# A chunked recurrence with two expert layers on one Trainium2 core: the triangular inverse in two interleaved streams, its solve on four 32x32 tiles, and later loads of the first layer's weights

## The chip, the cores and the metric

One core of a Trainium2 chip runs the whole program. The metric is the device time of one execution in microseconds. The kernel before takes 1128.68 us (median of 3 runs, 1117.59 to 1130.25).

## The reference, cut to what matters

```python
for t in range(S):                                   # S = 768 steps, 4 batches x 8 heads, D = 40
    y[:, :, t] = np.einsum('bhd,bhde->bhe', rt, state)
    Sa = np.einsum('bhde,bhe->bhd', state, at)
    state = state * wt[:, :, None, :] - np.einsum('bhd,bhe->bhde', Sa, bt)
    state = state + np.einsum('bhd,bhe->bhde', vt, kt)
x = y as 3072 tokens x 320
x = leaky(x @ w_in) @ w_out                          # 320 -> 2048 -> 320
out = (sigmoid(x @ w_gate) * (x @ w_val)) @ w_out2   # 320 -> 1536 -> 320
```

All of it is float32. The steps of one head depend on each other, the heads don't.

## The kernel before, in words

**The recurrence.** The 768 steps are cut into chunks of L = 64. A unit is 2 chunks (c = 0, 1) of 16 heads; there are NU = 12 units, and 24 pairs n = 2u + c. Eight heads lie beside each other in the free dimension (q = 0 to 7) and two more on the two halves of the partitions (i = 0, 1). Inside a chunk the sequential part is a unit lower triangular system. Its 64x64 matrix is split at C = 32 into two diagonal 32x32 blocks and one 32x32 cross block. All 64 diagonal blocks of a unit are inverted at once on VectorE: they are written to DRAM (`store_p`), come back with one block to each partition in `p_unit` (`load_p_top`, `load_p_low`: rows 0 to 15 and 16 to 31; two half inverses of each block lie on 128 partitions), and `inverse_columns` builds the inverse in `t_unit` column by column. A column is one multiply (L1255, into `prod`) and one add (L1259), over t//2 + 1 rows by 31 - t elements; each waits for the one before by a semaphore. The inverse goes back over DRAM (`store_t`, `load_t`) into `t_sb`.

**A pair n on TensorE** (PE), with the engine that empties each result: `pe_rhs_begin/end` (right side; ScalarE, `act_rhs`), `pe_first` (L698, upper half of the solve: `t_sb` times `rhs_sb`, 16 matmuls of 32x32 by 40; ScalarE, `act_first`), `pe_cross` (L708, the upper half's part in the lower half; ScalarE, `act_cross`), `pe_a_ka` (L630, L636: the matrices of unit g + 2 and g + 1; `act_a`, which also copies the cross block into `p_cross`, and `dve_ka`), `pe_ut_u` (L744, L747), `pe_st` (L761, the new state; VectorE, `dve_st`), `pe_vrur`, `pe_y_begin_sn`, `pe_y_end`. `pe_first` and `pe_cross` use the tile positions of the upper half of each i only. `FILL` lists matmuls with no use (L897) that stand behind some of these steps in the first units; 56 of them stand ahead of the first `pe_first`.

**Order.** Nothing is scheduled by a planner: each engine runs a hand-written loop over windows g = -2, -1, 0, ... and steps s = 0 to 7; unit g is in its main part in window g. From g = 2, s = 2 on, step number m = 8g + s - 18 of the first expert layer stands in each s: `up_products(m)` (L811), `act_g`, `dve_g_low` (L1306) and `down_products(m - 1)` (L826 to L831). There are 96 such steps, and then 72 steps of the second layer (L861, L879 to L881), which have TensorE alone from about 650 us on. In each window VectorE works at 31 columns: of unit g + 1 columns 7 to 12 at s = 0, 13 to 19 at s = 3, 20 to 26 at s = 4, 27 to 30 at s = 5, and of unit g + 2 columns 0 to 6 at s = 7.

**Weights of layer 1** come in 8 pieces of 0.6 to 0.8 MB into four staging buffers: GpSimd issues them (`load_piece`), ScalarE rounds them (`split_hi`), VectorE computes what is left over (`split_lo`, L1332 to L1339). Pieces 0 to 3 are issued at the end of window -1. GpSimd's queue also holds the products of a, b, k with the decays (`pool_a`, `pool_b`, `pool_k`) and the fetches of the next a, b, k. SyncE's queue holds nearly all other transfers, in the order of `sync_program`.

## Time and profile before

| | |
|---|---|
| runs, us | 1117.59, 1128.68, 1130.25 |
| profiled execution, us | 1121.75 (span of the profile 1120.0) |
| busy share | TensorE 94%, weight loads 80%, VectorE 55%, ScalarE 35%, GpSimd 13% |
| mean granted clock of TensorE | 0.98 of full speed |
| chain that ended last | TensorE 83%, VectorE 7%, issue 4%, the rest 6% |

The span is the stretch from the first to the last instruction, and the profiled execution took 1.75 us more than it. A matmul that overlaps with its neighbours has a long record, so TensorE's busy share doesn't say how much it achieved; the starts of its instructions do. "Idle before" names what ended an engine's wait.

### The profile page before, as it was taken

The numbers are of one execution on the slowest core, as the hardware profiler recorded it, in microseconds if no ns is written. First come the engines' busy times: TensorE is split into PE (matmuls) and PEld (weight loads), VectorE is DVE, ScalarE is ACT, GpSimd is POOL, SyncE is SP. The second block draws the span as 40 slices with busy tenths as digits, with TensorE's granted clock in tenths as the row PEclk, the third lists the DMA queues.
The fourth block names the chain that finished last, engine by engine and source line by source line (L and its number), as shares of the span: only waits on it lengthen the run. The fifth ranks groups of instructions, "written<-read, shape, count | busy, mean of one in ns | idle before, by whom it ended". The sixth has DMA issues, their size and how long they took to land.

```text
span 1120.0 us, 36607 instructions
## 1 busy us (share of the span) xinstructions
PE 1053.4 (94%) x16106; PEld 897.1 (80%) x16106; DVE 612.3 (55%) x1330; ACT 397.6 (35%) x782; POOL 145.1 (13%) x179
## 2 busy tenths in 40 slices
PE   3887779999999999999999999999999999999998
PEld 2776668788787877787878788888888888888887
DVE  7788977768687777677664234343232232323222
ACT  2142334345344443433443345542222222222222
POOL 6313130312213130303000000000000000000000
PEclk9988979999999999999999999999999999999999
DMA  5936364343426342533433034230202002020000
GB/s 176 256 93 153 87 123 94 88 111 107 116 47 142 88 110 61 132 81 93 96 84 76 9 106 135 77 90 1 61 1 62 1 1 62 1 61 1 24 1 23
DMA packets 133857, 87.63 MB, mean 78 GB/s; under 512 B 98274, under 2 KB 113634, under 8 KB 133700
## 3 DMA queue, kind: packets, MB, share of 16 engines
q1 hardware_dynamic: 126740, 62.85, 23.1%
q0 software_dynamic: 6960, 22.45, 6.8%
q8 instruction: 127, 2.08, 0.8%
q14 instruction: 30, 0.25, 0.1%
HBM read 66.39 MB, written 18.87 MB: 76 GB/s over the span
## 4 chain that ended last, share of the span: by engine, by line
PE 83%; DVE 7%; issue 4%; ACT 2%; POOL 2%; DMA 1%; SPq 0%; ACTq 0%; DVEq 0%; POOLq 0%
PE bank L811 15%; PE bank L861 12%; PE pair L861 12%; PE bank L881 4%; PE bank L879 4%; PE bank L880 4%; PE bank L826 4%; PE bank L827 3%; PE bank L828 3%; DVE prod L1255 2%; DVE t_unit L1259 2%; PE bank L786 2%; PE bank L630 2%; PE bank L897 2%; PE bank L830 2%
## 5 line engine op out<-in xcount | busy, mean ns | idle before, releaser
L1306 DVE TENSOR_TENSOR g_lo<-g_full,g_hi 128x512 fp32r<-128x512 f32 x168 | 125.2, 745 | 208.9 <-ACT g_hi L1066 208.8
L1066 ACT CAST g_hi<-g_full 128x512 fp32r<-128x512 f32 x168 | 104.4, 621 | 135.0 <-DVE g_full L1359 132.0
L811 PE MATMUL bank<-x_hi,w_up 128*128 128x512 f32 x480 | 135.8, 413 | 0.4 <-issue 0.2
L1059 ACT ACTIVATE g_full<-bank 128x512 f32<-128x512 f32 x96 | 57.5, 599 | 197.2 <-PE bank L811 185.9
L1255 DVE TENSOR_TENSOR prod<-t_unit,p_unit 128x126 f32<-128x126 f32 (+22 forms) x372 | 99.5, 267 | 19.8 <-DMA p_unit<-p_dram 6.5
L1259 DVE TENSOR_TENSOR t_unit<-t_unit,prod 128x126 f32<-128x126 f32 (+22 forms) x372 | 102.2, 275 | 12.8
L811 PEld LDWEIGHTS bank<-x_hi,w_up 128*128 128x128 f32 x480 | 86.0, 190 | 19.7 <-issue 0.9
L1359 DVE TENSOR_TENSOR g_full<-pair,h_sb 128x512 f32<-128x512 f32 x36 | 24.9, 691 | 113.1 <-PE pair L861 112.4
L811 PE MATMUL bank<-x_lo,w_up 128*128 128x512 f32 x288 | 82.0, 393 | 0.0
L826 PE MATMUL bank<-g_hi,w_dn 128*128 128x512 f32 x192 | 77.2, 402 | 2.9 <-DVE g_lo L1306 2.9
L1359 DVE TENSOR_TENSOR g_full<-bank,h_sb 128x512 f32<-128x512 f32 x36 | 24.9, 691 | 94.3 <-PE bank L861 86.3
L827 PE MATMUL bank<-g_hi,w_dn 128*128 128x512 f32 x192 | 75.1, 391 | 0.0
L828 PE MATMUL bank<-g_lo,w_dn 128*128 128x512 f32 x192 | 74.9, 390 | 0.0
L811 PEld LDWEIGHTS bank<-x_lo,w_up 128*128 128x128 f32 x288 | 54.7, 190 | 12.3
L861 PE MATMUL bank<-x_hi,up 128*128 128x512 f32 x240 | 62.8, 391 | 0.0
L861 PE MATMUL pair<-x_hi,up 128*128 128x512 f32 x240 | 62.8, 391 | 0.0
L630 PE MATMUL bank<-a_sb,b_sb 40*64 40x64 f32 x768 | 34.2, 252 | 28.2 <-POOL a_sb L301 24.9
L881 PE MATMUL bank<-dn,g_lo 128*128 128x320 f32 x192 | 59.3, 309 | 0.0
L880 PE MATMUL bank<-dn,g_hi 128*128 128x320 f32 x192 | 59.3, 309 | 0.0
L879 PE MATMUL bank<-dn,g_hi 128*128 128x320 f32 x192 | 59.1, 308 | 0.0
L630 PEld LDWEIGHTS bank<-a_sb,b_sb 40*64 40x64 f32 x768 | 30.7, 163 | 30.6 <-issue 26.1
L861 PEld LDWEIGHTS bank<-x_hi,up 128*128 128x128 f32 x240 | 44.1, 188 | 7.9
(149 smaller groups left out, 2410.7 us busy)
## 6 DMA issues: line engine op xcount, KB each, us to landing
p_unit<-p_dram SPq DMA_DIRECT2D x48, 128.0 KB, 2.9
stage<-in_w_out POOLq DMA_DIRECT2D x7, 640.0 KB, 5.0
v_tok<-in_vT SPq DMA_DIRECT2D x12, 320.0 KB, 3.2
v_nu<-in_vN SPq DMA_DIRECT2D x24, 160.0 KB, 5.6
x<-y_sb SPq DMA_DIRECT2D x48, 80.0 KB
k_sb<-in_kF POOLq DMA_DIRECT2D x22, 160.0 KB, 3.4
v_sb<-in_vF SPq DMA_DIRECT2D x22, 160.0 KB
r_sb<-in_rF SPq DMA_DIRECT2D x22, 160.0 KB
```

What stands on the lines that cost most here:

```text
L811: last = nc.tensor.matmul(up_bank(m)[:], lhs, rhs, start=(e == 0), stop=(e == len(products) - 1))
L826: nc.tensor.matmul(bank[1 + kk][:], w_high, hi, start=(f == 0), stop=False)
L827: nc.tensor.matmul(bank[1 + kk][:], w_low, hi, start=False, stop=False)
L828: nc.tensor.matmul(bank[1 + kk][:], w_high, lo, start=False, stop=(f == NF1 - 1))
L861: last = nc.tensor.matmul(o[:], lhs, rhs, start=(x == 0), stop=(x == len(products) - 1))
L879: nc.tensor.matmul(o, g_hi[:, par, tok], wt[:, 0, f % GT], start=(f == 0), stop=False)
L880: nc.tensor.matmul(o, g_hi[:, par, tok], wt[:, 1, f % GT], start=False, stop=False)
L881: last = nc.tensor.matmul(o, g_lo[:, par, tok], wt[:, 0, f % GT], start=False, stop=(f == NF2 - 1))
L1066: nc.scalar.copy(g_hi[:, m % 2], g_full[:]).then_inc(g_hi_ready, 1)
L1255: nc.vector.tensor_tensor(terms, t_unit[:, 0:m, t:t + 1].to_broadcast([P, m, rest]), p_unit[:, t, t + 1:C].unsqueeze(1).to_broadcast([P, m ...
L1259: nc.vector.tensor_tensor(t_unit[:, 0:m, t + 1:C], t_unit[:, 0:m, t + 1:C], terms, ALU.add).then_inc(column_ready, 1)
L1306: nc.vector.tensor_tensor(g_lo[:, m % 2], g_full[:], g_hi[:, m % 2].bitcast(F32), ALU.subtract).then_inc(g_lo_ready, 1)
```

## The change

It has seven parts.

- `inverse_columns` handles a column as two streams, the even and the odd rows of `t_unit`, each with its own semaphores: multiply even, multiply odd, add even, add odd. `columns_done` waits for both.
- From g = 2 on the columns of unit g + 1 lie otherwise: 7 to 10 at s = 0, 11 to 13 at s = 2, 14 to 19 at s = 3; the rest as before.
- `pe_first` writes heads q < 4 to the upper and q >= 4 to the lower quarter of each half, and `pe_cross` reads them there. The order of q is 0, 4, 1, 5, ..., so four 32x32 tile positions come in turn. `act_a` copies `p_cross` in four pieces in place of two.
- Pieces 0 to 3 of the weights are issued in window 0, behind `pool_a` of unit 2 and a wait for `t_loaded` of unit 0.
- `split_hi` of pieces 0 to 3 lies one step later in window 0 (s = 1 to 4), `split_lo` too (s = 3 to 6).
- SyncE issues `load_p_top(1)` ahead of `store_t(0)`.
- ScalarE runs `act_first` ahead of `act_x` in even windows.

```diff
@@ pool
+                if g == 0:
+                    pool.wait_ge(t_loaded, 64)
+                    for i in range(4):
+                        load_piece(pool, i)
                 if g == 1:
                     load_piece(pool, 6)
...
-                if g == -1:
-                    pool.wait_ge(p_low_loaded, 32)
-                    for i in range(4):
-                        load_piece(pool, i)
@@ SyncE
+            load_p_top(sp, 1)
             store_t(sp, 0)
-            load_p_top(sp, 1)
@@ TensorE, pe_first and pe_cross
-            for q in range(TQ):
+            for q in (x for low in range(HQ) for x in (low, low + HQ)):
                 for i in range(2):
-                    last = nc.tensor.matmul(o[upper(i), q * D:(q + 1) * D], t_sb[upper(i), c, q, 0:C],
+                    last = nc.tensor.matmul(o[first_rows(i, q), q * D:(q + 1) * D], t_sb[upper(i), c, q, 0:C],
                                             rhs_sb[upper(i), q], start=True, stop=True)
...
-                    last = nc.tensor.matmul(rhs_place(q)[lower(i)], p_cross[upper(i), u % 2, c, q],
-                                            u_first[upper(i), q], start=False, stop=True, skip_group_check=True)
+                    last = nc.tensor.matmul(rhs_place(q)[lower(i)], p_cross[first_rows(i, q), u % 2, c, q],
+                                            u_first[first_rows(i, q), q], start=False, stop=True,
+                                            skip_group_check=True)
@@ ScalarE
+                    if s == 1 and now:
+                        act_first(act, n)
                     if s == (0 if g == NU else 1) and g % 2 == 0 and 2 <= g // 2 <= NJ:
                         act_x(act, g // 2 - 1)
...
-                    if g == 0 and s < 4:
-                        split_hi(act, s)
+                    if g == 0 and 1 <= s <= 4:
+                        split_hi(act, s - 1)
@@ VectorE, inverse_columns
+                for e in range(min(m, 2)):
+                    rows = (m + 1 - e) // 2
+                    terms = prod[:, 80 * e:80 * e + rows * rest].rearrange("p (r t) -> p r t", t=rest)
+                    streams.append((e, rows, terms))
+                for e, rows, terms in streams:
+                    wait(dve, column_ready[e], done[e])
+                    nc.vector.tensor_tensor(terms, t_unit[:, e:m:2, t:t + 1].to_broadcast([P, rows, rest]),
+                                            p_unit[:, t, t + 1:C].unsqueeze(1).to_broadcast([P, rows, rest]), ALU.mult
+                                            ).then_inc(column_multiplied[e], 1)
+                for e, rows, terms in streams:
+                    dve.wait_ge(column_multiplied[e], done[e] + 1)
+                    nc.vector.tensor_tensor(t_unit[:, e:m:2, t + 1:C], t_unit[:, e:m:2, t + 1:C], terms, ALU.add
+                                            ).then_inc(column_ready[e], 1)
@@ VectorE, vector_program
-                        inverse_columns(dve, g + 1, 7, 13)
+                        inverse_columns(dve, g + 1, 7, 11 if g >= 2 else 13)
+                    elif s == 2 and soon and g >= 2:
+                        inverse_columns(dve, g + 1, 11, 14)
                     elif s == 3 and soon:
-                        inverse_columns(dve, g + 1, 13, 20)
+                        inverse_columns(dve, g + 1, 14 if g >= 2 else 13, 20)
...
-                    if g == 0 and 2 <= s <= 5:
-                        split_lo(dve, s - 2)
+                    if g == 0 and 3 <= s <= 6:
+                        split_lo(dve, s - 3)
```

The order on VectorE in a window from g = 2 on, from the decay of step 1 to the first columns of step 3 (`u_first` and `st_sb` are the state's update, `x_f` the two results of `pe_vrur`; a row ends with partitions x elements). Before:

```order
L1240 SCALAR_TENSOR_TENSOR inv<-w_raw,restart 128x520
L1306 TENSOR_TENSOR g_lo<-g_full,g_hi 128x512
L1275 TENSOR_TENSOR u_first<-pair,st_sb 128x320
L1278 TENSOR_TENSOR st_sb<-u_first,decay 128x320
L1288 TENSOR_TENSOR x_f<-bank,mask 128x512 x2
L1255 TENSOR_TENSOR prod<-t_unit,p_unit 128x126
L1259 TENSOR_TENSOR t_unit<-t_unit,prod 128x7x18
L1255 TENSOR_TENSOR prod<-t_unit,p_unit 128x136
L1259 TENSOR_TENSOR t_unit<-t_unit,prod 128x8x17
```

And now:

```order
L1257 SCALAR_TENSOR_TENSOR inv<-w_raw,restart 128x520
L1278 TENSOR_TENSOR prod<-t_unit,p_unit 128x60 x2
L1283 TENSOR_TENSOR t_unit<-t_unit,prod 128x3x20 x2
L1278 TENSOR_TENSOR prod<-t_unit,p_unit 128x76
L1278 TENSOR_TENSOR prod<-t_unit,p_unit 128x57
L1283 TENSOR_TENSOR t_unit<-t_unit,prod 128x4x19
L1283 TENSOR_TENSOR t_unit<-t_unit,prod 128x3x19
L1278 TENSOR_TENSOR prod<-t_unit,p_unit 128x72
L1278 TENSOR_TENSOR prod<-t_unit,p_unit 128x54
L1283 TENSOR_TENSOR t_unit<-t_unit,prod 128x4x18
L1283 TENSOR_TENSOR t_unit<-t_unit,prod 128x3x18
L1330 TENSOR_TENSOR g_lo<-g_full,g_hi 128x512
```

Columns 11 to 13 (elements 20, 19 and 18 long) have moved ahead of `g_lo`, and each column has four rows where it had two.

GpSimd's queue from the last products of window -1 on. Before:

```order
L301 TENSOR_TENSOR a_sb<-a_sb,decay 128x512
L329 DMA stage<-in_w_in 128x1536
L331 DMA stage<-in_w_out 128x1280
L329 DMA stage<-in_w_in 128x1536 x2
L438 DMA k_sb<-in_kF 40x1024 x2
L429 DMA b_sb<-in_bF 40x1024 x2
L321 TENSOR_TENSOR k_sb<-k_sb,inv 128x512
L311 TENSOR_TENSOR b_sb<-b_sb,inv 128x512
L301 TENSOR_TENSOR a_sb<-a_sb,decay 128x512
L420 DMA a_sb<-in_aF 40x512 x2
```

And now:

```order
L307 TENSOR_TENSOR a_sb<-a_sb,decay 128x512
L444 DMA k_sb<-in_kF 40x1024 x2
L435 DMA b_sb<-in_bF 40x1024 x2
L327 TENSOR_TENSOR k_sb<-k_sb,inv 128x512
L317 TENSOR_TENSOR b_sb<-b_sb,inv 128x512
L307 TENSOR_TENSOR a_sb<-a_sb,decay 128x512
L335 DMA stage<-in_w_in 128x1536
L337 DMA stage<-in_w_out 128x1280
L335 DMA stage<-in_w_in 128x1536 x2
L426 DMA a_sb<-in_aF 40x512 x2
```

The four weight loads have moved behind the fetches of k and b and three products, and the fetch of a now stands behind them.

ScalarE in an even window from g = 4 on, step 1. Before:

```order
L1066 CAST g_hi<-g_full 128x512
L1076 CAST x_hi<-x_f 128x512 x3
L1023 COPY u_first<-bank 128x320
L1030 COPY rhs_sb<-pair 128x160 x2
L981 ACTIVATE p_sb<-bank 128x512
L983 ACTIVATE p_cross<-bank 32x256 x2
```

And now:

```order
L1082 CAST g_hi<-g_full 128x512
L1039 COPY u_first<-bank 128x320
L1092 CAST x_hi<-x_f 128x512 x3
L1046 COPY rhs_sb<-pair 128x160 x2
L994 ACTIVATE p_sb<-bank 128x512
L997 ACTIVATE p_cross<-bank 32x128 x4
```

The copy that `pe_cross` waits for has moved ahead of three casts, and `p_cross` is written in four copies of half the size.

## Rows read from the trace of the kernel before

**Rows 1.** Four stretches: us, busy time of each engine, PEclk, DMA share, GB/s

```profile
25.00:55.00 30.00, 25.27 (x404) 24.29 (x404) 21.35 (x78) 6.15 (x14) 10.17 (x14) 1.00 0.92 256
55.00:65.00 10.00, 9.78 (x207) 9.08 (x208) 7.18 (x21) 3.53 (x10) 0.00 (x0) 0.52 0.08 23
...
100.00:150.00 50.00, 37.25 (x1131) 33.16 (x1130) 43.93 (x105) 16.47 (x35) 14.14 (x18) 0.84 0.61 133
...
200.00:300.00 100.00, 97.72 (x2260) 80.24 (x2254) 75.39 (x184) 43.86 (x95) 20.47 (x26) 1.00 0.43 103
```

**Rows 2.** The chain that ended last, near the first solve: start us, us, what

```profile
37.19 14.90 PE bank L897 x112
52.09 3.13 issue
55.22 1.15 PE bank L698 x32
```

**Rows 3.** SyncE's issues, 29 to 52 us: start us, us, line, transfer

```profile
28.97 15.33 SPq L477 DMA_DIRECT2D p_dram<-p_sb  x8
44.34 3.07 SPq L504 DMA_DIRECT2D t_dram<-t_unit  x2
...
49.97 2.17 SPq L515 DMA_DIRECT2D t_sb<-t_dram  x4
```

**Rows 4.** Transfers issued from 25 to 60 us: size, us from issue to landing

```profile
stage<-in_w_in POOLq DMA_DIRECT2D x3, 768.0 KB, 13.6
...
t_dram<-t_unit SPq DMA_DIRECT2D x2, 128.0 KB, 4.8
t_sb<-t_dram SPq DMA_DIRECT2D x4, 64.0 KB, 3.5
```

**Rows 5.** VectorE, two dependent instructions of the inverse of unit 0

```profile
36.10 0.29 DVE L1255 TENSOR_TENSOR prod<-t_unit,p_unit 128x126 f32<-128x126 f32 x1
36.43 0.29 DVE L1259 TENSOR_TENSOR t_unit<-t_unit,prod 128x126 f32<-128x126 f32 x1
```

**Rows 6.** VectorE, neighbours of which neither waits for the other

```profile
68.15 1.27 DVE L1288 TENSOR_TENSOR x_f<-bank,mask 128x512 f32<-128x512 f32 x2
...
75.94 1.39 DVE L1299 TENSOR_TENSOR y_sb<-bank,decay 64x512 f32<-64x512 f32 x2
...
77.70 1.22 DVE L1339 TENSOR_TENSOR w_dn<-stage,w_dn 128x1024 fp32r<-128x1024 f32 x1
78.84 0.28 DVE L1255 TENSOR_TENSOR prod<-t_unit,p_unit 128x121 f32<-128x121 f32 x1
```

**Rows 7.** VectorE, the state updates of pairs 0, 1, 2 and 3

```profile
66.37 0.49 DVE L1275 TENSOR_TENSOR u_first<-pair,st_sb 128x320 f32<-128x320 f32 x1 [0.97 <-PE pair L761]
...
87.13 0.49 DVE L1275 TENSOR_TENSOR u_first<-pair,st_sb 128x320 f32<-128x320 f32 x1
...
112.84 0.49 DVE L1275 TENSOR_TENSOR u_first<-pair,st_sb 128x320 f32<-128x320 f32 x1 [2.02 <-PE pair L761]
...
131.36 0.49 DVE L1275 TENSOR_TENSOR u_first<-pair,st_sb 128x320 f32<-128x320 f32 x1
```

**Rows 8.** TensorE in windows 6 and 7: start us, us, line, matmul, idle before

```profile
353.88 0.76 PE L698 MATMUL bank<-rhs_sb,t_sb 32*32 32x40 f32 x32
354.57 0.50 PE L826 MATMUL bank<-g_hi,w_dn 128*128 128x512 f32 x1
...
359.17 0.42 PE L630 MATMUL bank<-a_sb,b_sb 40*64 40x64 f32 x3 [0.86 <-POOL a_sb L301]
...
411.09 0.27 PE L630 MATMUL bank<-a_sb,b_sb 40*64 40x64 f32 x2
...
412.07 0.23 PE L744 MATMUL pair<-t_sb,rhs_sb 64*40 64x64 f32 x2
```

**Rows 9.** Waits over the whole span: us in total, times, longest

```profile
PE pair L708 <- ACT u_first L1023: 3.1, 4, 1.1
...
PE bank L826 <- DVE g_lo L1306: 2.9, 3, 1.0
```

More of the change, by code:

```diff
@@ L105, in rwkv_mlp_kernel @@
         t_unit = sb(ctx, "t_unit", [P, C // 2, C])
-        prod = sb(ctx, "prod", [P, 136])
+        prod = sb(ctx, "prod", [P, 152])
         def vrur(i):
@@ L160, in rwkv_mlp_kernel @@
         diagonal_set = sem("diagonal_set")
-        column_multiplied = sem("column_multiplied")
-        column_ready = sem("column_ready")
+        column_multiplied = [sem(f"column_multiplied{i}") for i in range(2)]
+        column_ready = [sem(f"column_ready{i}") for i in range(2)]
         t_stored = sem("t_stored")
@@ L202, in lower, with first_rows @@
             return slice(L * i + C, L * i + 2 * C)
+        HQ = TQ // 2
+        def first_rows(i, q):
+            return upper(i) if q < HQ else lower(i)
         def wait(engine, signal, value):
@@ L488, in load_p_top @@
                 if u > 0:
-                    sp.wait_ge(column_ready, (C - 1) * (u - 1) + C // 2)
+                    columns_done(sp, u - 1, C // 2)
                 load_p_rows(sp, slice(0, C // 2), p_top_loaded)
@@ L493, in load_p_low, with columns_done @@
             if unit_in(u):
-                wait(sp, column_ready, (C - 1) * u)
+                if u > 0:
+                    columns_done(sp, u - 1, C - 1)
                 load_p_rows(sp, slice(C // 2, C), p_low_loaded)
+        def columns_done(engine, u, t):
+            wait(engine, column_ready[0], (C - 1) * u + t)
+            wait(engine, column_ready[1], (C - 3) * u + t - 2)
         def store_t(sp, u):
             if unit_in(u):
-                sp.wait_ge(column_ready, (C - 1) * (u + 1))
+                columns_done(sp, u, C - 1)
                 wait(sp, t_loaded, 64 * u)
@@ L705, in pe_cross @@
             emptied(pe, "first", n)
-            for q in range(TQ):
+            for q in (x for low in range(HQ) for x in (low, low + HQ)):
                 for i in range(2):
-                    last = nc.tensor.matmul(rhs_place(q)[lower(i)], p_cross[upper(i), u % 2, c, q],
-                                            u_first[upper(i), q], start=False, stop=True, skip_group_check=True)
+                    last = nc.tensor.matmul(rhs_place(q)[lower(i)], p_cross[first_rows(i, q), u % 2, c, q],
+                                            u_first[first_rows(i, q), q], start=False, stop=True,
+                                            skip_group_check=True)
             last.then_inc(cross_multiplied, 1)
@@ L982, in act_a @@
             for i in range(2):
-                last = nc.scalar.mul(p_cross[upper(i), u % 2, c], src[upper(i), :, C:L], -1.0)
+                for q in (0, HQ):
+                    last = nc.scalar.mul(p_cross[first_rows(i, q), u % 2, c, q:q + HQ],
+                                         src[upper(i), q:q + HQ, C:L], -1.0)
             last.then_inc(bank_emptied[bank_of("a", n)], 1)
@@ L992, in act_t_unit @@
             wait(act, t_stored, 32 * u)
-            wait(act, column_ready, (C - 1) * u)
+            if u > 0:
+                columns_done(act, u - 1, C - 1)
             nc.scalar.copy(t_unit[:].rearrange("p r t -> p (r t)"), restart[:, 1:2].to_broadcast([P, C // 2 * C])
@@ L1139, in scalar_program @@
                         act_g(act, m)
+                    now, soon, later = unit_in(g), unit_in(g + 1), unit_in(g + 2)
+                    if s == 1 and now:
+                        act_first(act, n)
                     if s == (0 if g == NU else 1) and g % 2 == 0 and 2 <= g // 2 <= NJ:
                         act_x(act, g // 2 - 1)
-                    now, soon, later = unit_in(g), unit_in(g + 1), unit_in(g + 2)
                     if s == 0 and now:
@@ L1146, in scalar_program @@
                         if now:
-                            act_first(act, n)
                             act_cross(act, n)
@@ L1252, in inverse_columns @@
                 m, rest = t // 2 + 1, C - 1 - t
-                terms = prod[:, 0:m * rest].rearrange("p (r t) -> p r t", t=rest)
-                wait(dve, column_ready, (C - 1) * u + t)
-                nc.vector.tensor_tensor(terms, t_unit[:, 0:m, t:t + 1].to_broadcast([P, m, rest]),
-                                        p_unit[:, t, t + 1:C].unsqueeze(1).to_broadcast([P, m, rest]), ALU.mult
-                                        ).then_inc(column_multiplied, 1)
-                dve.wait_ge(column_multiplied, (C - 1) * u + t + 1)
-                nc.vector.tensor_tensor(t_unit[:, 0:m, t + 1:C], t_unit[:, 0:m, t + 1:C], terms, ALU.add
-                                        ).then_inc(column_ready, 1)
+                done = ((C - 1) * u + t, (C - 3) * u + t - 2)
+                streams = []
+                for e in range(min(m, 2)):
[11 more added lines that the diff above has]
+                                            ).then_inc(column_ready[e], 1)
         def dve_ka(dve, n):
```

## The prediction, as it was put on record before the changed kernel ran

> **What bounds the kernel now.** I read the windows first: between 200 and 300 us TensorE has matmuls running for 97.72 of 100 us [rows 1]. From the first expert layer on, only less TensorE time or fewer of its waits can help. The prologue ahead of it is another matter, so I read the chain there. In it TensorE runs 56 useless matmuls from 37.19 to 52.09, waits 3.13 us, and starts the first solve at 55.22 [rows 2]. What it waits for is the inverse of unit 0. SyncE's issues show how it comes: it is stored from 44.34 and loaded from 49.97, and one batch of eight small stores ahead of it took 15.33 us to issue [rows 3]. The transfers of that stretch tell why: the DMA engines are 92% busy at 256 GB/s [rows 1] while the weight pieces take 13.6 us to land, a store of the inverse 4.8 and its load 3.5 [rows 4]. Right behind the wait the granted clock falls to 0.52 [rows 1], that is from 2.4 GHz to the lower level of 1.2. After that the prologue is paced by VectorE: the state updates of pairs 0 and 1 start 20.8 us apart, those of pairs 2 and 3 18.5 us, and those of pairs 1 and 3 wait for nothing but VectorE's own queue [rows 7].
>
> **Two streams in a column.** Two dependent instructions of 126 elements start 0.33 us apart with 0.29 of work [rows 5]. 1024 elements take 1.22 [rows 6], so an element costs (1.22 - 0.29) / 898 = 1.04 ns, an instruction 0.16 on top, and a dependent successor starts 0.20 plus the elements later. A successor that waits for nothing starts earlier: 1.14 after the 1024 elements (0.08 above their 1.06), and two of 512 take 1.27 together, so the second starts 0.58 after the first (0.05 above 0.53) [rows 6]. A column of 126 costs 2 x 0.33 = 0.66 now. As four instructions of 63 it costs the larger of 4 x (0.066 + 0.08) = 0.58 (the engine) and 2 x (0.066 + 0.20) = 0.53 (the dependence). Short columns gain less; I take 0.075 on each of 29 columns, 2.2 us a unit. Best case, with 0.05 for a start, the dependence rules: 3.5 us gained. Worst case, each instruction pays 0.16 + 0.03 as two neighbours on different halves do (1.39 for two of 64x512, no overlap [rows 6]): 1.02 for that column and about 0.32 lost on each, +9.2 us a unit. I take the middle one since L1255 behind L1339 is the very instruction, with its semaphore already counted up.
>
> The Trainium skill has rules for both sides (VectorE: DVE Perf Modes). Its section "The DRAIN you can't avoid" says that the next operation starts only when the pipe has emptied, and advises few operations, which speaks against this change; the section "Two Vector instructions with no wait between them" says that only neighbours whose operands start in other groups of 32 partitions are held. The rows bear out the second: the overlap is in rows 6, and the pair without one is the pair on two halves. By the first rule the sum would be the slow rival below.
>
> **The start, unit 0.** The store of its inverse is issued at 44.34 [rows 3]; with 2.2 less, 42. Without weights in flight I take 4 us for the store and 4.5 for four issues and the load (landings of 4.8 and 3.5 were under load [rows 4]): 50.5. The useless matmuls last until 52.09, so they cover it by 1.6 us and no more than 3.1 can be had: **-3.1** (bounds 0 and -3.1). The clock: from 55.22 to the state update at 66.37 [rows 2, 7] pass 11.15 us, with solve, filler, `pe_a_ka` and `pe_ut_u` at 1.2 GHz (a solve lasts 1.15 [rows 2], at full clock 0.76 [rows 8]). I assume that without the idle 3.13 us the clock stays up. TensorE's 10 us then become 6, but behind `pe_a_ka` VectorE still has `ka_sb` and a decay (512 elements and two scans of 520 with small steps between, some 3.5 us by my estimate), so 7.5 remain: **-3.7** (bounds 0 and -4.5).
>
> The weights now go out at about 50.5. Landing in 13.6 at worst [rows 4] they are there by 65; rounding them starts behind `pe_ut_u` of pair 0, at about 59, with piece 0, which was issued first. Behind them in GpSimd's queue stand the fetch of a for pair 5 and its product, needed by `pe_a_ka` some 8.5 us after the first state update, near 68: covered by 2 to 3 us. If it is not, that is 2 to 4 us (in the second rival).
>
> **VectorE's stretches.** Between pairs 0 and 1 stand 18 columns (-1.3) and three splits; the third (1024 and 512 elements, so 1.2 + 0.7 us) moves behind the update. That is **-3.1** of 20.8. The row of pair 1 shows no wait for TensorE [rows 7], so it is not next at once; how far ahead it is the row can't tell, which is the near end of the bounds. Between pairs 2 and 3 only the columns are shorter: **-1.3** (bounds for both together: -3.0 and -6.5; with held streams +8). Moving the last split costs nothing: the update of pair 2 comes 25.7 us after that of pair 1 [rows 7], set by the transfers of b and v.
>
> **Steady part, windows 2 to 11.** The solve: 16 matmuls (32 records) take from 353.88 to 354.57, 0.69 us, 0.13 of it to drain: 18 ns a record with two tile positions in use. `pe_a_ka` has four in use: 64 records in 412.07 - 411.09 = 0.98 us, 15 ns each [rows 8]. At 15 a solve takes 0.58, saving 0.11. If tile time alone counted, it would be 18 x 2 / 4 = 9 ns, 0.41 us, saving 0.28. Nearest is `pe_a_ka`; 40 products (`pe_first` and `pe_cross` of 20 pairs) x 0.11 = **-4.4** (bounds 0 and -11). The first four pairs lie in the prologue and count as nothing. The two more copies of `p_cross` cost ScalarE about 0.3 us a pair beside `up_products`: nothing.
>
> Here the skill has an objection (TensorEngine Tiling (Array Packing), "Gotcha 1: PSUM Pressure"): tiles in different rows can't write one PSUM bank at once. `pe_first` writes one bank from both halves of the rows. But so does `pe_a_ka`, at 15 ns [rows 8]; by the rule `pe_first` would save nothing and the sum would be 2.2 higher.
>
> ScalarE's order: `pe_cross` waited for `u_first` 4 times, 3.1 us in all [rows 9], behind three casts of `act_x`. The copy is now first, and the casts lie beside `down_products`. In window 6 `pe_a_ka` waits for GpSimd right after (0.86 [rows 8]), and that wait grows by what is gained: **-2.2** (bounds -1 and -4.5, the latter if a short dip of the clock that follows goes too). VectorE's order: `down_products` waited for `g_lo` three times, 2.9 us [rows 9], behind the six columns of s = 0. Four shorter ones (2.3 us by the sum above against 3.9) end 1.6 us earlier: **-2.9** (bounds -1.5 and -3). The three columns that come ahead of `g_lo` at s = 2 cost 1.7 us where VectorE has some 0.7 idle, but `down_products` needs `g_lo` only a step later.
>
> **The sum.** -3.1 - 3.7 - 3.1 - 1.3 - 4.4 - 2.2 - 2.9 = -20.7. The profiled execution took 1121.75 (span 1120.0), so 1101. It lies 6.9 us under the median of the runs shown, and executions scatter by 13 us; for a median I add 2: **1103 us**.
>
> **The rivals.**
> - *The prologue keeps its price.* The clock falls all the same, since a gap of another cause is enough, or the weights collide with the fetch of a. For it speaks that 100 to 150 us, with many short waits and filler too, ran at 0.84 [rows 1]; against it, that 25 to 55 us ran at 1.00 [rows 1], filler included. The 3.7 is lost and 2 to 4 come on top: 1109.
> - *Four tiles run at tile speed* (9 ns): 6.7 more, and with the dip gone 2 more: 1094. Against it: `pe_a_ka` has the same 40 elements or more to a record in four tiles and stays at 15 [rows 8].
> - *The tiles gain nothing* and all else holds: 1107.
> - *VectorE is held between the streams*: +9.2 us a unit. At unit 0 it is 7 beyond the 1.6 us of cover, +5.7 in each of two VectorE stretches where I had -1.3, and in ten steady windows VectorE goes from about 40 busy us in 53 to 49, which delays `g_lo` and the update by 1 to 2 us a window. Against the forecast's 1103 that is 11 + 7 + 7 + about 15: 1143, slower than before. It decides as soon as a column of 126 takes over 0.75 us.
>
> **Chances.** Forecast 0.45, prologue keeps its price 0.24, tile speed 0.16, no gain of the tiles 0.10, held 0.05. The range leaves out the last and the outer ends: 1088 to 1118. A difference of 2% is about what a measurement of this kernel can tell from none; below the median of before it is 1106.1. The forecast lies just beyond it and counts 0.3 of its 0.45, tile speed 0.15, the others 0.07: faster 0.52, within 2% 0.44, slower 0.04.
>
> **What would show it.** Right: no wait between filler and first solve and a clock of 1.00 from 55 to 65; updates of pairs 0 and 1 near 59 and 77 us, of pairs 2 and 3 17 us apart; the first `up_products` some 11 us sooner than before; columns of 0.58 us; a solve of 0.58; the two waits of rows 9 gone. Wrong: starts of neighbours in two streams a full duration apart; a new wait of ScalarE for `stage`, of GpSimd for a, or of TensorE for `g_lo` in step 3.

## The result and the profile after

The changed kernel takes 1108.53 us in the median (1102.66 to 1116.55, four executions) beside 1123.2 us for the kernel before: a ratio of 0.9863, 95% interval 0.9815 to 0.9912. Timed again with a later batch it gives 1110.04 and 0.9853 (0.9808 to 0.9899). The ratios and their intervals leave out executions over 1.5% above the fastest of the same kernel. The changed kernel is faster, by 14 to 15 us or 1.4%, which is clear of the scatter and under 2%; the forecast of 1103 is about 6 us too low. The profiled execution took 1112.1 us (span 1110.3). The stages are not where I had them. Starts in us, read from the timelines of both traces:

| | before | after, forecast | after |
|---|---|---|---|
| first solve | 55.22 | 52.1 | 52.29 |
| state update of pair 0 | 66.37 | 59 | 64.26 |
| of pair 1 | 87.13 | 77 | 81.86 |
| of pair 2 | 112.84 | | 110.07 |
| of pair 3 | 131.36 | | 129.90 |
| first `up_products` | 155.45 | some 11 sooner | 153.78 |
| first gate product | 723.9 | | 714.2 |
| end of the span | 1120.0 | | 1110.3 |

So the prologue gained 1.7 us and not 11.2; the steady part gained 8.0 (568.4 to 560.4), about what I had (-9.5). One trace is one execution: the changed kernel's second trace has 54.51 for the first solve, 66.01, 84.90, 111.68 and 131.61 for the updates, 153.90 for the first `up_products` and 711.65 for the gate product, 557.8 us later. Six traces (the two of the changed kernel and experiments 1, 4, 6 and 10) have the same code from 160 us on, and take 557.2 to 563.2 us over the steady part. So a difference of under 6 us there, between two traces, shows little. Two windows that answer to [rows 1], with the same columns:

```profile
55.00:65.00 10.00, 5.93 (x180) 5.44 (x176) 5.99 (x13) 5.45 (x10) 2.94 (x3) 0.70 0.83 301
...
100.00:150.00 50.00, 41.91 (x1212) 38.16 (x1212) 41.90 (x151) 16.72 (x37) 14.93 (x20) 0.74 0.56 136
```

Between 55 and 65 us TensorE is busy for 5.93 us of 10, the DMA engines for 83% (8% before), and the clock stands at 0.70, not 1.00. The chain of work through that stretch says what happened (start us, us, what; the chain of [rows 2]):

```profile
43.98 8.38 PE bank L910 x75
52.36 0.42 PE bank L710 x32
...
56.45 4.07 issue
```

The wait of 3.13 us ahead of the first solve is gone, and the solve (now L710) takes 0.42 us. But 57 matmul records into the 64 of `pe_ut_u` (L757, L760) TensorE stands for 4.07 us, and the chain can only call it "issue": no semaphore released it. The DMA view for 58 to 60 us shows what arrives then (queue, kind: packets, MB, share):

```profile
q0 software_dynamic: 148, 0.81, 99.1%
q8 instruction: 1, 0.02, 3.0%
```

One packet of 16 KB comes on the instruction queue, beside 0.81 MB of GpSimd's transfers: the weight pieces, which are now issued here. GpSimd's queue in the timeline of after (in brackets the idle time before, and what ended it):

```profile
51.74 0.61 POOL L335 DMA_DIRECT2D stage<-in_w_in  x1 [3.89 <-DMA t_sb<-t_dram]
...
53.92 1.05 POOL L426 DMA_DIRECT2D a_sb<-in_aF  x2
...
64.43 1.18 POOL L307 TENSOR_TENSOR a_sb<-a_sb,decay 128x512 f32<-128x512 f32 x1 [2.73 <-DMA a_sb<-in_aF]
```

The gain on SyncE is as large as it looked. Without weights in flight its batch of eight stores takes 6.46 us to issue where it took 15.33 [rows 3]:

```profile
28.97 6.46 SPq L483 DMA_DIRECT2D p_dram<-p_sb  x8
...
42.65 1.27 SPq L516 DMA_DIRECT2D t_dram<-t_unit  x2
```

VectorE's columns, for [rows 5] (here two instructions of 63 elements in one row, "x2"):

```profile
30.89 0.36 DVE L1278 TENSOR_TENSOR prod<-t_unit,p_unit 128x63 f32<-128x63 f32 x2
...
31.43 0.35 DVE L1278 TENSOR_TENSOR prod<-t_unit,p_unit 128x60 f32<-128x60 f32 x2
```

A column of 126 elements starts at 30.89 and the next at 31.43: 0.54 us, where it was 0.66. The state updates of pairs 0 and 2, for [rows 7], and TensorE's waits from 160 to 712 us, for [rows 9] (us in all, times, longest):

```profile
64.26 0.49 DVE L1299 TENSOR_TENSOR u_first<-pair,st_sb 128x320 f32<-128x320 f32 x1 [3.87 <-PE pair L774]
...
110.07 0.49 DVE L1299 TENSOR_TENSOR u_first<-pair,st_sb 128x320 f32<-128x320 f32 x1 [3.47 <-PE pair L774]
```

```profile
PE pair L757 <- issue: 3.7, 3, 1.5
PE bank L642 <- POOL a_sb L307: 3.1, 2, 2.3
PE bank L710 <- issue: 2.2, 3, 1.0
PE bank L824 <- issue: 2.1, 2, 1.2
PE pair L760 <- issue: 2.0, 1, 2.0
```

The same stretch of the kernel before, where the two waits of [rows 9] stand ahead of these:

```profile
PE pair L744 <- issue: 2.2, 2, 1.5
PE pair L747 <- issue: 1.7, 1, 1.7
PE bank L698 <- issue: 1.5, 3, 1.0
PE bank L630 <- POOL a_sb L301: 0.9, 1, 0.9
```

In after both are gone, as forecast. Yet the lists add up to 13.1 us after and, with the 6.0 of [rows 9], 12.3 before: the 6.0 us came back, 2.2 as a longer wait for GpSimd's a and 4.6 as "issue" (5.4 before, 10.0 after). In the six traces with the same code from 160 us on, "issue" is 8.0 to 13.1 us (8.5 in the changed kernel's second trace), so its growth is clear and its size isn't.

### The profile page after: what moved, and what is told of

The parts are those of the page before. It is cut to its first block, busy times and chain, and to the rows that moved or that the text cites. A ratio compares the mean times of both kernels' runs of the same rounds, so it can differ in the third digit from the quotient of the medians.

```text
span 1110.3 us, 37363 instructions
## 1 busy us (share of the span) xinstructions
PE 1046.9 (94%) x16106; PEld 889.8 (80%) x16106; DVE 617.0 (56%) x2026; ACT 406.4 (37%) x830; POOL 142.9 (13%) x179
## 4 chain that ended last, share of the span: by engine, by line
PE 88%; issue 4%; DMA 3%; DVE 2%; POOL 2%; SPq 1%; ACT 1%; ACTq 0%; POOLq 0%; DVEq 0%
PE bank L824 17%; PE bank L874 12%; PE pair L874 12%; PE bank L839 4%; PE bank L840 4%; PE bank L841 4%; PE bank L894 4%; PE bank L892 4%; PE bank L893 4%; PE bank L910 2%; PE bank L799 2%; PE bank L843 2%; PE bank L844 2%; PE bank L786 2%; PE bank L642 2%
## 5 line engine op out<-in xcount | busy, mean ns | idle before, releaser
L1330 DVE TENSOR_TENSOR g_lo<-g_full,g_hi 128x512 fp32r<-128x512 f32 x168 | 120.7, 718 | 216.6 <-ACT g_hi L1082 216.4
L1278 DVE TENSOR_TENSOR prod<-t_unit,p_unit 128x31 f32<-128x31 f32 (+4 forms) x720 | 131.1, 222 | 5.4 <-ACT t_unit L1016 3.2
L1283 DVE TENSOR_TENSOR t_unit<-t_unit,prod 128x31 f32<-128x31 f32 (+4 forms) x720 | 132.8, 224 | 0.8
L1383 DVE TENSOR_TENSOR g_full<-pair,h_sb 128x512 f32<-128x512 f32 x36 | 24.9, 692 | 112.7 <-PE pair L874 112.0
L1383 DVE TENSOR_TENSOR g_full<-bank,h_sb 128x512 f32<-128x512 f32 x36 | 24.9, 692 | 94.6 <-PE bank L874 86.3
L874 PEld LDWEIGHTS pair<-x_hi,up 128*128 128x128 f32 x240 | 44.1, 188 | 7.9
```

Of the source, the lines that this page charges most:

```text
L874: last = nc.tensor.matmul(o[:], lhs, rhs, start=(x == 0), stop=(x == len(products) - 1))
L1278: nc.vector.tensor_tensor(terms, t_unit[:, e:m:2, t:t + 1].to_broadcast([P, rows, rest]), p_unit[:, t, t + 1:C].unsqueeze(1).to_broadcast( ...
L1283: nc.vector.tensor_tensor(t_unit[:, e:m:2, t + 1:C], t_unit[:, e:m:2, t + 1:C], terms, ALU.add).then_inc(column_ready[e], 1)
L1330: nc.vector.tensor_tensor(g_lo[:, m % 2], g_full[:], g_hi[:, m % 2].bitcast(F32), ALU.subtract).then_inc(g_lo_ready, 1)
```

## The experiments

Two questions: what holds TensorE in `pe_ut_u` of pair 0 (theory A: the fetch of its own instructions, delayed by the weight transfers; theory B: TensorE has become too fast for that fetch), and which part gains what. The runs came in three batches, each on another chip and with its own runs of the kernel before; the ratios below are to those. In the quoted expectations S2 is the state update of pair 2.

**1. The weight pieces where they were (`w_early`).**

```
-                if g == 0:
-                    pool.wait_ge(t_loaded, 64)
-                    for i in range(4):
-                        load_piece(pool, i)
...
+                if g == -1:
+                    pool.wait_ge(p_low_loaded, 32)
+                    for i in range(4):
+                        load_piece(pool, i)
```

> The changed kernel with only the four weight pieces asked for where the kernel before did (end of window -1). Theory A: TensorE's 4.3 us of idle time in pe_ut_u of pair 0, in which a packet of the instruction queue comes, is the fetch of its instructions held up by the weight transfers that the change puts there. Then under 1 us of it is left, the state update of pair 0 comes near 61.5 instead of 64.3 (a wait of 0 to 2 us before the first solve is back), and the kernel takes 1105 to 1108 us against the changed kernel's 1108.5. Theory B: the fetch is late because TensorE now runs through its instructions faster there, whatever the DMA engines carry. Then 3 to 4.5 us of idle time stay, and with the wait before the solve the kernel takes 1108 to 1112.

Measured: 1118.46 us, ratio 0.995 (0.9909 to 0.999), 1% above the changed kernel. The idle time in `pe_ut_u` is gone, but the first solve comes at 58.35, 6 us later than after and 3 later than before, and right at it the clock is at the lower level, so TensorE went through its instructions at half speed and theory B would have none either. The run doesn't tell A from B. It bears on the worth of the move: everything of the change but the weights' place gives 0.5%, with it 1.4%. The traces show less of it: the first `up_products` stand at 155.07, 1.2 to 1.3 us behind the changed kernel's two, and the profiled execution took 1110.15 us. SyncE in this run:

```profile
29.83 14.40 SPq L483 DMA_DIRECT2D p_dram<-p_sb  x8
48.98 1.12 SPq L487 DMA_DIRECT2D p_unit<-p_dram  x2
50.20 1.27 SPq L516 DMA_DIRECT2D t_dram<-t_unit  x2
```

The batch takes 14.4 us again, and `load_p_top(1)`, now ahead of the store, waits for its landing. So the store of the inverse leaves at 50.20, where it left at 44.34 before, and part of what this run lacks is the price of the new order on SyncE. Whether that order gains anything when the weights are out of the way, no run shows.

**2. Four tiles alone, and 3. two streams alone, on the kernel before.** The first takes `pe_first`, `pe_cross` and the copies of `p_cross` from the change, the second `inverse_columns` and its semaphores.

> The kernel before with only the four-tile solve (pe_first, pe_cross, the copies of p_cross). A solve takes 0.42 us as in the changed kernel's trace. Theory 1 (the saving of 0.27 us a product reaches the end): 40 x 0.27 = 10.8 us less, 1112 against 1123. Theory 2 (part of it comes back as a wait of pe_a_ka for GpSimd's product of a right behind it): that wait grows from 0.9 to 3 to 5 us in all and 5 to 8 us are gained, 1115 to 1118.

> The kernel before with only the inverse's columns in two streams. A column of 126 elements takes 0.54 instead of 0.65 us. Theory 1: only the prologue gains, about 2.2 us at unit 0 and 1.3 in each VectorE stretch: the wait before the first solve is near 1 us, and the first up_products come 4 to 5 us sooner, 1118 to 1119 in all. Theory 2 (the clock or another wait takes it back): first up_products within 1.5 us of before and 1122 to 1124. In the steady part both expect 0 to 1 us (down_products waits less for g_lo).

Four tiles: 1116.85 us, 0.9953 (0.9914 to 0.9992). Two streams: 1115.19 us, 0.9949 (0.9915 to 0.9982). Each is 5 to 6 us by its ratio. With four tiles a solve takes 0.42 us. From the first `up_products` to the gate layer it gains only 3.7 of the 10.8 us (568.4 to 564.7), and the rest isn't in the wait that I named: that for a stays at 0.9 us, while others grow:

```profile
PE pair L714 <- ACT u_first L1032: 4.6, 4, 1.7
PE pair L751 <- issue: 3.5, 3, 1.7
PE bank L833 <- DVE g_lo L1315: 3.4, 4, 1.3
PE bank L704 <- issue: 2.1, 3, 1.2
...
```

The copy of `u_first` from 3.1 to 4.6, g_lo from 2.9 to 3.4, "issue" from 5.4 to 8.2. The streams did the reverse of what I expected. Unit 0 gained nothing: the last column was done near 42 us, but SyncE was still in its batch, which ended at 44.7:

```profile
29.19 15.53 SPq L477 DMA_DIRECT2D p_dram<-p_sb  x8
44.83 3.13 SPq L510 DMA_DIRECT2D t_dram<-t_unit  x2
```

The first solve comes at 55.56. The gain lies in the steady part, 5.5 us (562.9), where the wait for g_lo goes altogether, its columns being shorter. Its first `up_products` come 2.0 us sooner.

**4. The fetch of a ahead of the weights (`fetch_first`).** GpSimd's `fetch_a(pool, n + 5)` of window 0 stands ahead of the four pieces.

> The changed kernel with GpSimd's fetch of a for pair 5 issued ahead of the four weight pieces. GpSimd's wait of 2.73 us for it at 61.7 to 64.4 goes. If that wait set pe_a_ka of pair 1, the state update of pair 1 comes 1 to 2 us sooner; if the prologue is held by the late instructions and VectorE alone (my theory), nothing moves by over 0.5 us and the time is that of the changed kernel, 1108 to 1110. The 4.3 us of idle time in pe_ut_u of pair 0 stay in both.

1113.2 us, 0.9902 (0.9867 to 0.9936): nothing gained over the changed kernel. TensorE stands for 4.74 us in `pe_ut_u`. Pairs 0 and 1 are 17.4 us apart (17.6 after): GpSimd's wait had not been next. In this trace the first `up_products` come at 149.09, 4.7 us sooner than after, and 2.4 of that arise between pairs 2 and 3, where the clock is at 1.00; from the first `up_products` to the gate layer it takes 562.9 us.

**5. The changed kernel again, and 6. weights late (`w_late`).**

```
-                if g == 0:
-                    pool.wait_ge(t_loaded, 64)
-                    for i in range(4):
-                        load_piece(pool, i)
...
                     pool_a(pool, n + 5)
+                if g == 0:
+                    for i in range(4):
+                        load_piece(pool, i)
...
-                    if g == 0 and 1 <= s <= 4:
-                        split_hi(act, s - 1)
+                    if g == 0 and 3 <= s <= 6:
+                        split_hi(act, s - 3)
...
-                    if g == 0 and 3 <= s <= 6:
-                        split_lo(dve, s - 3)
+                    if g == 0 and 4 <= s <= 7:
+                        split_lo(dve, s - 4)
```

> The changed kernel itself, timed again beside the next three on one chip, since its first comparison had four executions. Expected 1108 to 1113 and a ratio of 0.986 to 0.991; its profile shows whether the 4 to 5 us of idle time in pe_ut_u of pair 0 comes in every execution (theory A and B both: yes).

> The changed kernel with the four weight pieces behind GpSimd's products of pair 5 (some 10 us later, near 63), and their rounding and splitting two and one steps later. So no weights fly while TensorE goes through the first solve and pe_ut_u at full clock. Theory A (the transfers hold up its instructions): the idle time in pe_ut_u of pair 0 falls from 4.3 to about 1.6 us, as in the trace of the four tiles alone, where no weights flew either; state update of pair 0 near 61, and 1 to 3 us in all are gained, 1106 to 1109 if the changed kernel is at 1110. Theory B (TensorE is simply too fast for its fetch, in the changed kernel the more as nothing slows it): 4 us stay. Both: the later splits may hold VectorE at pair 1 or 2 and give the gain back.

`w_late`: 1113.3 us, 0.9912 (0.9879 to 0.9945), nothing gained. Its trace settles the cause. The first solve starts at 51.86, TensorE runs at full clock, its instructions up to the 57th record of `pe_ut_u` come at the pace of the changed kernel, and the idle time there falls to 0.9 us. TensorE's waits in this stretch, `w_late` first, then the changed kernel run again, then experiment 8, which has the weights at the new place and the slower solve:

```profile
PE pair L755 <- issue: 0.9, 1, 0.9
```
```profile
PE pair L757 <- issue: 3.6, 1, 3.6
```
```profile
PE pair L756 <- issue: 4.2, 1, 4.2
```

With weights in flight it is 3.3 to 4.7 us in six traces (both of the changed kernel and experiments 4, 7, 8 and 10), at either speed of the solve; without them 0.9, and 1.4 in `four_tiles_only`, whose weights had landed. Theory A holds for some 3 us; the last 0.9 to 1.4 us stay without any weights, as B would have them. With the idle time the drop of the clock goes too (the windows' columns as above):

```profile
52.00:62.00 10.00, 8.88 (x316) 7.88 (x310) 9.86 (x47) 3.80 (x11) 1.35 (x2) 1.00 0.12 30
```

The state update of pair 0 comes at 60.42, near the forecast's 59. But the idle time has only moved with the weights. They are issued at 63.16 here, and 2 us later TensorE stands for its instructions in `pe_y_end` of pair 0 (L797):

```profile
65.35 3.13 issue
```

At this record seven other traces have 0.3 to 1.7 us, with at most 0.3 MB moved in the 4 us before its end, where `w_late` has 1.35. Another 1.51 us follow at 74.06, and the clock from 65 to 80 us is at 0.62 to 0.69. VectorE passes both waits on to pair 1:

```profile
DVE y_sb L1321 <- PE bank L797: 3.2, 1, 3.2
DVE ka_sb L1287 <- PE bank L646: 1.2, 1, 1.2
```

So pairs 0 and 1 are 20.4 us apart and not 17.6, although one split has left this stretch (-1.6 us). Then TensorE waits 2.57 us for instructions in `pe_kb` and 2.00 in `pe_st`, pair 2 comes at 112.70, and the 3.8 us are lost.

**7. GpSimd's product of a ahead of that of b (`a_before_b`).**

```
-                    pool_b(pool, n + 4)
-                    pool_a(pool, n + 4)
+                    for scale in (pool_a, pool_b) if g >= 1 else (pool_b, pool_a):
+                        scale(pool, n + 4)
```

and the same for n + 5.

> The changed kernel with GpSimd's product of a ahead of that of b from window 1 on. pe_a_ka waited 3.1 us in all for that product behind the faster solve, and a half-clock stretch of 6.8 us follows the longer one. Theory: the wait is the gain of the solve given back, and goes with the order: 3 to 5 us sooner from the first up_products to the gate layer, 0.997 of the changed kernel. Rival: the same 3 us come back as waits for instructions or for g_lo a little later, and the time is within 1 us of the changed kernel.

1113.38 us, 0.9909 (0.9878 to 0.994): nothing gained. The rival is nearer, though its 1 us is missed by the medians (3.3). The trace, of an execution of 1119.43 us, takes 567.5 us from the first `up_products` to the gate layer, where I had 3 to 5 us less than 560.4. From 160 to 712 us the wait for a is gone, one of 0.8 us for b is new, and "issue" stands with 13.9 us (these and ones of 1.7 and 0.4), where the two traces of the changed kernel have 10.0 and 8.5, and the six with its code up to 13.1:

```profile
PE pair L757 <- issue: 6.0, 4, 2.2
PE bank L824 <- issue: 3.6, 3, 1.3
PE bank L710 <- issue: 2.2, 3, 0.8
...
```

**8. Two tiles again (`two_tiles_again`).** The changed kernel with `pe_first`, `pe_cross` and `act_a` as before.

> The changed kernel with the solve on two tiles as before (18 ns a record). Theory 1 (each solve's 0.27 us counts where nothing else waits): 40 solves cost 10.8 us, less the waits that the faster solve brought (3.1 for a, some 4 more for instructions): 4 to 6 us slower than the changed kernel. Theory 2 (the tiles' gain goes wholly into those waits): within 1.5 us of it.

1118.4 us, 0.9942 (0.9908 to 0.9976) beside 0.9853 (0.9808 to 0.9899): by medians the tiles are worth 8 us here. The traces don't show them: the steady part takes 560.8 us here, and 560.4 and 557.8 in the changed kernel's two. The wait for a is back at 0.6 us (2.0 to 3.5 in the six traces with the changed kernel's code), so the faster solve did bring that one on.

**9. Shifted instructions (`shift`), 10. v sooner (`v_early`), 11. both.**

```
-            for _ in range(FILL.get((place, n), 0)):
-                nc.tensor.matmul(bank[0][:, 0:P], ident[:], ident[:], start=True, stop=True)
+            if (place, n) == ("sn", 0):
+                widths = [P] * 13 + [P // 2] * 86
+            else:
+                widths = [P] * FILL.get((place, n), 0)
+            for width in widths:
+                nc.tensor.matmul(bank[0][:, 0:width], ident[:], ident[:, 0:width], start=True, stop=True)
...
-                if u > 0 and unit_in(u + 2):
+                if u > 1 and unit_in(u + 2):
                     sp.wait_ge(b_fetched[u % 2], 32 * (u // 2 + 1))
```

and the same for the branch behind it, the wait for k.

> The changed kernel with 43 of the 56 useless matmuls of 128 columns cut into 86 of 64: the same columns, but 86 more matmul records, so every later instruction lies further along in the stream that TensorE fetches in blocks. Theory A (blocks of a fixed number of instructions, here some 126 matmul records, each asked for some 150 records ahead, which full clock runs through in 3 us, and the fetch takes 7 us beside the weights): the idle time in pe_ut_u of pair 0 at its 57th record goes, and one of 2 to 4 us comes in pe_st of pair 0 near its 25th; the state update of pair 0 comes near 62 instead of 64 to 66. Rival (the idle time belongs to what pe_ut_u reads or writes): it stays in pe_ut_u at the 57th record with 3.5 to 5 us.

> The changed kernel without SyncE's wait for b ahead of the v, r and v_nu loads of unit 1. In the changed kernel the chain to the state update of pair 2 goes over b (5.7 us) and only then v_nu (6.5 us) before pe_st. Theory 1: that chain is why S2 stands at 109 to 114 us however early pair 1 is; without it v_nu is there by 98, S2 comes 3 to 6 us sooner and 2 to 4 us are left at the end. Theory 2: b and k then share the DMA engines with v, land 3 to 5 us later, and S2 moves by under 1.5 us.

> Both edits of the two runs before. If both theories hold, S2 comes 4 to 7 us sooner than in the changed kernel and the time is 3 to 5 us under it, near 1106, the best version so far; if neither, within 1 us of it, 1109 to 1112.

`shift`: 1127.84 us, 1.0031 (0.9982 to 1.0079). `v_early`: 1112.88, 0.9922 (0.9886 to 0.9958). Both: 1120.15, 1.0001 (0.9966 to 1.0035). The trace of `shift` is of its slowest execution (1136.88 us), so I read the one of both. My edit had a flaw: a matmul of 64 columns takes nearly as long as one of 128 (the 99 take 24.9 us), so the first solve comes at 61.30 and not at 52. By then the weights have landed: their queue moves 0.07 MB from 62 to 64 us and nothing from 64 to 66, where `pe_ut_u` runs. Hence the 3 us that the transfers add can't show here, and only the 0.9 to 1.4 us that stay without weights can have moved. They did: at full clock `pe_ut_u` of pair 0 runs through without a stop, and the first wait for instructions stands in the solve of pair 1. From 60 to 76 us this is the only one:

```profile
PE bank L710 <- issue: 1.2, 1, 1.2
```

So the idle time doesn't belong to what `pe_ut_u` reads or writes, as the rival had it. No wait came at the forecast place (the 25th record of `pe_st`) either, with the weights landed. The surprise is the steady part, from 160 to 712 us:

```profile
PE pair L760 <- issue: 8.8, 3, 5.0
PE bank L824 <- issue: 6.1, 5, 1.8
PE bank L642 <- POOL a_sb L307: 3.3, 2, 2.1
...
```

With two more of 1.5 and 0.9 that is 17.3 us of "issue", where `v_early`, without the 86 records, has 10.5 and none of the twelve traces without them over 13.9 (`shift` has 21.0, in its slowest execution); from the first `up_products` to the gate layer it takes 567.5 us and `v_early` 563.2.

`v_early` alone did nothing, as theory 2 had it, though with another reason beside. The wait that I took away ended at 98.12 in the changed kernel, and SyncE issues the first v load at 97.58 without it, since it stands behind loads of p and w in its own queue; v_nu then takes 11.0 us to land and not 6.5. Pair 2 comes at 112.2.

**12. The orders alone (`orders_only`),** on the kernel before: `act_first` ahead of `act_x`, and the columns 11 to 13 at s = 2.

> The kernel before with only the two new orders: ScalarE's copy of u_first ahead of act_x, and VectorE's columns 11 to 13 moved from s = 0 to s = 2. My terms: 2.2 for the first and, of the 2.9 of the second, about 1.5, since the columns stay as long as before: 3 to 4 us sooner between the first up_products and the gate layer, 1118 to 1120 in all. Rival: pe_a_ka's wait for a grows by what is gained and g_lo waits in another step: 0 to 1 us. In both the prologue stays as before within 1.5 us.

1120.61 us, 1.0008 (0.9974 to 1.0042): no change, the rival is right. Both waits of [rows 9] are gone (6.0 us) and 568.2 us pass to the gate layer, 0.2 less than before. From 160 to 712 us:

```profile
PE pair L744 <- issue: 4.9, 3, 1.8
PE bank L630 <- POOL a_sb L301: 2.0, 1, 2.0
PE bank L698 <- issue: 1.9, 3, 0.7
...
```

With two more of 1.7 and 1.1 "issue" has 9.6 us for 5.4; the wait for a has 2.0 for 0.9. No version beat the changed kernel.

## Why the prediction was right and wrong

**In sum.** By parts the changes alone give 0.5% (four tiles), 0.5% (streams) and 0 (orders). All of them without the weights' move give 0.5% (`w_early`), with it 1.4%, so the parts don't add up. From one profiled execution to the other I had 20.7 us less, and the traces show 9.7: the prologue was taken for 9.5 us too much and the steady part for 1.5. In the steady part two errors went opposite ways: the solve was taken for 6.4 too little, and the two orders' 5.1 and 2.8 more didn't come. That the median is only 6 us off, and not 11, is luck: 2 us were added for a median, and the changed kernel's median lies 3.6 below its profiled execution.

**The start.** Right: the wait ahead of the first solve is gone (-2.9 of -3.1; the second trace has none either, with the solve at 54.51). The reason was half wrong. I had the store of the inverse leave sooner by the 2.2 us that the columns save; experiment 3 shows that the columns alone bring nothing there, as SyncE's batch ends at 44.7. It is the weights' absence that frees SyncE (6.46 us for the batch, 14.40 in `w_early`).

**The clock, -3.7.** Wrong, and so is the 59 for pair 0. From the first solve to the update pass 11.97 us, 0.8 more than before, where I had 7.5. The assumption "without the idle 3.13 us the clock stays up" is true by itself (`w_late`: 1.00 from 52 to 62, and 8.56 us for the stretch). The step that failed is the one before it: I priced the weights' new place by what waits for weights and by GpSimd's queue, and never asked what else flies on the DMA engines. TensorE's own instructions do. The rival "the prologue keeps its price" had the outcome ("a gap of another cause is enough") and the size, but its named collision, with the fetch of a, is not the cause (experiment 4).

**VectorE's stretches.** Pairs 0 to 1: 17.6 us, forecast 17.7. Right. Pairs 2 to 3: 19.8 instead of 17.2, and the clock goes with it. In the four traces with the two streams in which it stood at 0.90 to 1.00 over this stretch (experiments 1, 4, 6 and 8) it takes 17.3 to 17.4 us, as forecast; in the three with 0.57 to 0.71 (the changed kernel's two and experiment 10) 19.8 to 19.9, and VectorE waits 2.2 us there for `pe_y_end`. Between them I had put nothing, and 25.7 became 28.2. The chain from pair 1 to pair 2 shows where, in the kernel before and after:

```profile
91.86 1.19 issue
...
104.44 6.08 DMA v_nu<-in_vN
...
111.20 1.14 issue
```
```profile
86.59 2.02 issue
...
100.21 6.45 DMA v_nu<-in_vN
...
107.34 2.24 issue
```

Two waits for instructions lie in it, in `pe_kb` and `pe_st`, and grow by 0.8 and 1.1 us. Between them lies the path of the transfers: b takes 5.7 us to land in both traces, v_nu 6.1 and 6.5. Why these two waits grew isn't settled.

**The columns, 0.58 us.** The dependence bound, 0.53, was the right one (0.54 measured); the rival in which VectorE is held is out. (Its sum was short: at unit 0 it loses 2.2 + 9.2 = 11.4 us against the forecast, 9.8 beyond the cover and not 7.)

**The solve, 0.58 us.** Wrong; the tile-speed rival's 0.41 was right (0.42), against the nearest row, `pe_a_ka`'s 15 ns a record. A solve has 32 records of 32x40, `pe_a_ka` 64 of 40x64, with more rows and columns to a tile: the nearest row was of another shape. So the raw saving is 40 x 0.27 = 10.8 us, not 4.4. The sum had a slip too: 32 x 15 ns and 0.13 to drain are 0.61, not 0.58, and the term -3.2. The Trainium skill's objection (TensorEngine Tiling (Array Packing), "Gotcha 1: PSUM Pressure") doesn't show: `pe_first` writes one bank from both row halves, and still it went from 0.69 to 0.42 us.

**The two orders, -2.2 and -2.9.** The waits went; the gain didn't come. In the steady part the changed kernel has 10.8 (solves) + 6.0 (both waits) - 2.2 (a) - 4.6 (issue) = 10.0 us less, and the trace shows 8.0. Between 355 and 363 us the clock is at 0.57 instead of 0.79, which may take a part of the rest; 2 us are also less than what traces of the same code differ by. I foresaw the growth of the wait for a and left out "issue", which has 5.4 us in the kernel before from 160 to 712 us.

**What "issue" is.** It is a wait for TensorE's own instructions, and three things show it. It has fixed places in the stream. Counted in the traces' records of TensorE's matmuls, twelve traces have 16106 of them. Most of their stops up to 115 us stand after 725 records (the place in `pe_ut_u`), 977 (`pe_y_end`), 1102, 1228, 1355, 1481, 1607 and 1859, that is, some 126 apart or a multiple of it. The two traces with 86 records more stop after 1104, 1230, 1355, 1482 and 1608: at nearly the same numbers, but at instructions that lie 86 records further on. The DMA queue of instructions has one packet of 16 KB for about as many records (16106 / 127 = 126.8), in the pages of the changed kernel and of `shift`:

```profile
q8 instruction: 127, 2.08, 0.8%
```
```profile
q8 instruction: 128, 2.10, 0.8%
```

And the wait ends with such a packet: in the eight traces that stop after record 725 TensorE goes on 1.2 to 1.6 us after the packet has ended. With weights in flight (six traces) the packet starts 5.2 to 6.5 us after the first solve, without them (`w_late`, `four_tiles_only`) 2.6 to 2.7. The packet itself takes no longer beside them (0.96 us in the changed kernel, 0.95 in `w_late`), so it is its start that is late.

The steady part is less clear. The reading that fits is that a wait for data gives the fetch of instructions time to catch up, and when the wait is taken away, the fetch is next; traces of the same code differ by up to 5 us of "issue". The Trainium skill says (Runtime: NRT & Kernel Launch, section "Instruction fetch mechanics") that each engine fetches its instructions over a DMA queue of its own in blocks of 16 KiB, which agrees with the packets, and that the cost is mostly hidden. Here it isn't: 4.07 us at one place and 10.0 in the steady part. Why the packet starts late beside the weights, and whether it waits behind data packets inside a DMA engine, wasn't shown.

## What to carry to other kernels

When transfers are moved, list everything else that the DMA engines then carry, the instructions of a dense TensorE stretch among them: look in the list of waits for "issue" and in the DMA view for the instruction queue at the new time. Where a list of waits has "issue" beside the wait to be removed, expect part or all of the gain to turn up there; an edit that takes away 6 us of waits alone was worth nothing here. Moving the transfers again can move the wait with them, as `w_late` did. For a small matmul take the price from a row with the same tile shape, and time each part of a change alone before it is credited. Before two traces are compared by stage, see how far two traces of the same code lie apart.

## What the runs showed that I had not expected

- TensorE stood 3.3 to 4.7 us for its instructions with 2.9 MB of weights in flight, and 0.9 to 1.4 at the same place without. With the weights 11 us later it stood 3.13 us at a later place.
- Forty-three more matmuls at the start, which pushed the later instructions along, went with 17.3 us of "issue" 100 us and more later, where twelve traces without them have 5.4 to 13.9. That the places in the stream make the difference is likely; two traces don't prove it.
- A matmul of 64 columns took nearly as long as one of 128 (99 matmuls, 86 of them of 64 columns, took 24.9 us; 56 of 128 columns took 14.9).
- SyncE took 14.4 to 15.5 us to issue eight stores of 32 KB beside the weights, and 6.5 without them.
